# From expert output to first projections: copies, squares and first step in halves, stacks in number order

## The chip, the cores and the metric

The kernel runs on one core of a Trainium2 chip. The metric is device time in microseconds for one execution; the median of three runs of the kernel before is 797.98 us (796.89 to 799.02). The engines are TensorE (PE; its weight loads are listed as PEld), VectorE (DVE), ScalarE (ACT), GpSimd (POOL) and SyncE (SP), which here issues nearly all DMAs. Each works through its own queue in order, and they wait for each other on semaphores.

## The reference

Three layers follow each other: attention with pooled queries, a soft mixture of experts over the 2304 tokens, and a gated feed-forward layer with an RMS norm.

```python
# layer 2: 8 experts of 4 slots (n_slots = 32)
logits = x @ phi
slot_input = (softmax of logits over tokens).T @ x
for e in range(E):
    slot_out[e] = np.maximum(slot_input[e] @ w1[e], 0.0) @ w2[e]
c = softmax of logits over slots
x = c @ slot_out                                   # (2304, 512)
# layer 3, d_ff = 1536
rms = np.sqrt(np.mean(x * x, axis=-1, keepdims=True) + 1e-06)
xn = x / rms * rms_g
g = xn @ w_gate
out = (g * (1.0 / (1.0 + np.exp(-g))) * (xn @ w_val)) @ w_out
```

## The kernel before

The span of 794.3 us falls into attention (to about 545 us), the experts (to about 597 us), a short change-over (to about 619 us) and the last layer (to the end). The change lies in the change-over, and in the end of each of the two expert groups.

**Why there is a change-over.** The output of layer 2 has rank 32: each token is a mix `c` of 32 slot outputs. So the kernel never forms x. It multiplies the 32 slot outputs (scaled by rms_g) with w_gate and w_val once, to two 32 x 1536 matrices, and projects tokens from their 32 shares. A token's square sum is found from the 32 x 32 Gram matrix of the slot outputs.

**The expert output.** For each of two groups of four experts (loop over `g`), the second products gather in the bank `o_ps`; ACT copies the 128 x 512 result to `so_sb` (L1638, `o_out`), and PE transposes it in four pieces (`slot_transposes`, L1448). Two matmuls that only keep PE at work (`keep_clock`, L1432) are queued between them for the last group. DVE makes `st_plain` (L1757) and `st_scaled` (L1761); PE makes the Gram matrix.

**The squares.** PE multiplies the Gram matrix with the transposed shares `comb_t`: 512 columns (L1559) and 64 columns (L1560), then one signal `yt_ready`. DVE multiplies the 576 columns with `comb_t` into `product` (L1774). PE has `share(0, 1)` between, and then sums over slots in five pieces of 128 tokens (L1564, ten records). DVE scales to the mean (L1777), ACT takes the root (L1666), DVE the reciprocal `tok_a` (L1779).

**Shares and projections.** Tokens lie in five chunks: four of 512 and one of 256 (four tails of 64). `prescale(n)` (L1267) multiplies the shares of a chunk with `tok_a`; chunks 0 and 1 are made by DVE (`PROD_BY_DVE = 2`), 2, 3 and 4 by POOL. `share_transposes(n)` (PE, L1281) transposes four tiles of it into a PSUM bank, `shares_high(n)` (ACT, L1287) writes the rounded high part to `plain_t`, and `shares_low(n)` (DVE, L1292) subtracts it on the rows of the low part. `share(m, c)` (PE, L1515) is one quarter of slot outputs times w_gate (m = 0) or w_val (m = 1), and waits for the DMA of that quarter. After four quarters `high_half(m)` (ACT, L1655) and `low_half(m)` (DVE, L1770) split the result, and eight stacks `stack_share(k)` (PE, two matmuls, L1530 and L1532; k = 0 to 3 gate, 4 to 7 value) put it in a form of 128 rows. Two PSUM banks alternate between stacks; `share_out(k)` copies one out, 384 columns, on DVE (L1784) for k = 0, 4, 3 and on ACT (L1651) for the others. The stacks are issued in the order 0, 1, 4, 5, 2, 3, 6, 7. A projection is one matmul of 512 columns, `gate(n, f)` (L1541) or `value(n, f)` (L1545).

**The last layer.** It has 5 chunks x 12 tiles of d_ff = 60 steps. In a step, ACT takes Silu of the gate bank (L1663), DVE multiplies it with the value bank (`hid2`, L1813), ACT rounds that to `h_hi` (L1710), DVE takes the rest `h_lo` (L1818), and PE, after the projections of two steps ahead, issues 12 matmuls of 512 columns (L1617). In the first steps ACT also rounds w_out (`wo_high`, L1646) and POOL makes its low part (L1737), after it made the first high part itself (L1728).

**What sets the order.** The order on each engine is written out by hand: PE's list of `share`, `share_transposes`, `stack_share`, `gate` and `value` calls ahead of the step loop, ACT's and DVE's lists ahead of theirs. On ACT, one Silu of a single element (`warm`, L1669) after `shares_high(0)` loads the Silu table early. On SP the DMAs of w_gate, w_val and w_out are issued in this order right behind those of the experts' weights; no wait of SP stands on anything in the change-over.

Of the kernel before, what the change touches and what calls it, by code (L numbers as in the profile page):

```python
# [7 lines left out]
P = 128  # L8
FP32 = mybir.dt.float32
# [921 lines left out]
def rest(nc, mem, att, w_gate, w_val, w_out, out):  # L931
# [320 lines left out]
    prod_done, prod_rest, ct_ready = sem("prod_done"), sem("prod_rest"), sem("ct_ready")  # L1252
# [4 lines left out]
    PROD_BY_DVE = 2  # L1257

    def prescale(ops, n):
# [7 lines left out]
        return ops.tensor_tensor(dst, src.unsqueeze(2).broadcast_to(shape),  # L1267
                                 inv.unsqueeze(2).unsqueeze(3).broadcast_to(shape), ALU.mult)

    def share_transposes(pe, n):  # L1270

        bank = CT_BANK[n]
        if n < PROD_BY_DVE:
            pe.wait_ge(prod_done, n + 1)
        else:
            pe.wait_ge(prod_rest, n + 1 - PROD_BY_DVE)
# [53 lines left out]
    yt_ps = banks[:, 2:4, :]  # L1330
# [15 lines left out]
    used, stored = sem("used"), sem("stored")  # L1346
    SHARES = [(m, j) for m in range(2) for j in range(4)]
# [18 lines left out]
    PIECES_BY_DVE = (0, 4, 3)  # L1366

    def pieces_out(place):
        by_dve = sum(k in PIECES_BY_DVE for k in STACK_ORDER[:place + 1])
        return by_dve, place + 1 - by_dve  # L1370
# [53 lines left out]
    def _(pe):  # L1424
# [18 lines left out]
        def slot_transposes(g):  # L1443
            pe.wait_ge(o_out, g + 1)
            if g:
                pe.wait_ge(st_out, g)
            for c in range(KT):
                last = nc.tensor.transpose(st_ps[:, P * c:P * c + P], so_sb[:, P * c:P * c + P], ident[:])  # L1448
            last.then_inc(st_ready, 1)

        for g in range(NG):
# [31 lines left out]
            if g:  # L1483
                pe.wait_ge(o_out, g)
# [36 lines left out]
        def stack_share(k):  # L1521
# [3 lines left out]
            if stack_place(k) >= 2:  # L1525
                by_dve, by_act = pieces_out(stack_place(k) - 2)
                pe.wait_ge(wl_out_v, by_dve)
                if by_act:
                    pe.wait_ge(wl_out_a, by_act)
# [29 lines left out]
        nc.tensor.matmul(yt_ps[:, 0, :], gram[:], comb_t[:, 0:N], start=True, stop=True)  # L1559
        nc.tensor.matmul(yt_ps[:, 1, 0:TAIL], gram[:], comb_t[:, N:SQ], start=True, stop=True).then_inc(yt_ready, 1)  # L1560
        share(0, 1)
        pe.wait_ge(product_done, 1)
        for i in range(NI):
# [61 lines left out]
    def _(act):  # L1625
# [292 lines left out]
```

## Time and profile before

| | us |
|---|---|
| median of 3 runs (lowest to highest) | 797.98 (796.89 to 799.02) |
| the profiled execution | 796.09 |
| its span, from first to last instruction | 794.3 |
| PE busy | 777.4 (98%) |
| DVE busy | 465.2 (59%) |
| ACT busy | 461.8 (58%) |
| POOL busy | 182.0 (23%) |
| granted TensorE clock, mean | 0.998 of full |

The profile is of one execution, and all times in it are counted from the start of its span. PE's instructions are pipelined: the next starts before the one ahead has ended, so the text reckons a matmul's cost on PE from start to next start, and its delay for others from its start to the start of what waits for it. The same holds, by a smaller overlap, for ACT and DVE.

### The profile page before, as it was taken

To read this page: it belongs to the slowest core of one execution; us is meant where nothing else is said; L and a number is where in the kernel's file an instruction comes from. 1 tells how busy PE (TensorE), PEld (TensorE's weight loads), DVE (VectorE), ACT (ScalarE), POOL (GpSimd) and SP (SyncE) were. 2 spreads that over 40 slices of the span, in tenths; PEclk is the share of its full clock that TensorE was granted. 3 is DMA by queue.
4 is the path that set the end of the run, shared out by engine and by line. 5 is a ranking of instruction groups with operands and counts; after the bars stand their busy time and mean duration, and the time that the engine had idled before them with its cause. 6 is when DMAs were issued, how large, how long until landed. Compare 5 with 4: busy or idle time off the path is not lost.

```text
span 794.3 us, 16113 instructions
## 1 busy us (share of the span) xinstructions
PE 777.4 (98%) x5255; PEld 581.0 (73%) x5255; DVE 465.2 (59%) x895; ACT 461.8 (58%) x871; POOL 182.0 (23%) x244
## 2 busy tenths in 40 slices
PE   7999999999999999999999999999988999999998
PEld 7777777777777777777777777667324788888886
DVE  6767667666676666766666666654414545454443
ACT  5767676766767676767676676653104644343433
POOL 5351431513315233152241421000003420000000
PEclk9999999999999999999999999999999999999999
DMA  8539746374473653836538335949999001010101
GB/s 228 130 80 282 211 120 161 80 177 100 108 177 76 163 110 98 192 72 152 119 89 208 73 77 131 339 135 360 347 392 401 10 1 54 0 54 1 54 40 40
DMA packets 83030, 112.01 MB, mean 141 GB/s; under 512 B 45360, under 2 KB 47408, under 8 KB 82480
## 3 DMA queue, kind: packets, MB, share of 16 engines
q1 hardware_dynamic: 82832, 111.24, 49.3%
q8 instruction: 24, 0.39, 0.2%
q10 hardware_dynamic: 160, 0.26, 0.1%
q14 instruction: 14, 0.11, 0.0%
HBM read 71.37 MB, written 4.72 MB: 96 GB/s over the span
## 4 chain that ended last, share of the span: by engine, by line
PE 89%; SPq 4%; DMA 3%; POOL 2%; DVE 1%; issue 1%; ACT 0%; POOLq 0%; DVEq 0%; ACTq 0%
PE banks L521 23%; PE banks L584 20%; PE banks L617 19%; PE banks L1617 18%; SPq L1398 2%; PE banks L1541 2%; DMA weights<-in_moe_w 2%; PE banks L1545 2%; PE banks L1063 1%; DMA q_in<-in_q 1%; PE banks L1117 1%; PE banks L1082 1%; PE banks L1515 0%; PE banks L1468 0%; SPq L322 0%
## 5 line engine op out<-in xcount | busy, mean ns | idle before, releaser
L584 PE MATMUL banks<-k_stack,q_stack 128*128 128x384 f32 x960 | 274.8, 376 | 2.5 <-DVE q_stack L801 2.0
L772 ACT COPY pt<-banks 128x384 f32<-128x384 f32 x288 | 138.3, 480 | 152.9 <-PE banks L521 152.8
L521 PE MATMUL banks<-ident,probs 128*128 128x128 f32 x1296 | 219.6, 278 | 0.4 <-ACT probs L744 0.3
L521 PEld LDWEIGHTS banks<-ident,probs 128*128 128x128 f32 x1296 | 156.5, 140 | 67.7 <-issue 42.0
L744 ACT ACTIVATE probs<-banks,neg_max 128x1152 f32<-128x1152 f32 x144 | 175.9, 1222 | 7.4 <-DVE neg_max L841 3.0
L617 PE MATMUL banks<-pt,v_in 128*64 128x320 f32 (+1 forms) x1152 | 167.3, 417 | 0.9 <-ACT o_t L759 0.9
L584 PEld LDWEIGHTS banks<-k_stack,q_stack 128*128 128x128 f32 x960 | 147.4, 191 | 3.4 <-ACT k_stack L388 2.2
L837 DVE TENSOR_REDUCE row_max<-banks 128x1 f32<-128x384 f32 x144 | 80.1, 556 | 117.0 <-PE banks L584 115.4
L830 DVE TENSOR_REDUCE row_max<-banks 128x1 f32<-128x768 f32 x144 | 136.7, 949 | 1.7 <-PE banks L584 1.1
L617 PEld LDWEIGHTS banks<-pt,v_in 128*64 128x64 f32 x1152 | 72.0, 136 | 58.2 <-issue 25.9
L892 DVE COPY pt<-banks 128x384 f32<-128x384 f32 x144 | 80.3, 558 | 37.0 <-PE banks L521 34.3
L353 POOL TENSOR_TENSOR k_hi<-k_lo,one 128x512 fp32r<-128x512 f32 (+1 forms) x45 | 37.1, 826 | 279.7 <-ACT k_lo L690 262.3
L1617 PE MATMUL banks<-wo_hi,h_hi 128*128 128x512 f32 x216 | 84.5, 391 | 0.2 <-DVE h_lo L1818 0.2
L1617 PE MATMUL banks<-wo_lo,h_hi 128*128 128x512 f32 x216 | 84.2, 390 | 0.0
L1617 PE MATMUL banks<-wo_hi,h_lo 128*128 128x512 f32 x216 | 84.1, 389 | 0.0
L1813 DVE TENSOR_TENSOR hid<-silu,banks 128x512 f32<-128x512 f32 (+1 forms) x60 | 38.0, 633 | 40.7 <-ACT silu L1663 40.1
L1818 DVE TENSOR_TENSOR h_lo<-hid,h_hi 128x512 fp32r<-128x512 f32 (+1 forms) x60 | 38.4, 639 | 38.1 <-ACT h_hi L1710 38.1
L1710 ACT CAST h_hi<-hid 128x512 fp32r<-128x512 f32 (+1 forms) x60 | 34.7, 578 | 42.9 <-DVE hid L1813 42.9
L1663 ACT ACTIVATE silu<-banks 128x512 f32<-128x512 f32 (+1 forms) x60 | 33.3, 554 | 38.6 <-PE banks L1541 38.6
L1617 PEld LDWEIGHTS banks<-wo_hi,h_hi 128*128 128x128 f32 x216 | 40.5, 188 | 9.0 <-issue 0.7
L1617 PEld LDWEIGHTS banks<-wo_hi,h_lo 128*128 128x128 f32 x216 | 40.6, 188 | 8.5
L1617 PEld LDWEIGHTS banks<-wo_lo,h_hi 128*128 128x128 f32 x216 | 40.6, 188 | 7.9
(188 smaller groups left out, 663.3 us busy)
## 6 DMA issues: line engine op xcount, KB each, us to landing
weights<-in_moe_w SPq DMA_DIRECT2D x7, 2048.0 KB, 11.4
v_in<-in_v SPq DMA_DIRECT2D x16, 576.0 KB, 4.0
k_in<-in_k SPq DMA_DIRECT2D x30, 288.0 KB, 4.9
k_stack<-k_hi SPq DMA_DIRECT2D x30, 288.0 KB, 3.6
k_stack<-k_lo SPq DMA_DIRECT2D x30, 288.0 KB, 3.5
q_in<-in_q SPq DMA_DIRECT2D x14, 512.0 KB, 4.9
slots_of_four<-in_moe_w SPq DMA_DIRECT2D x12, 512.0 KB, 10.8
q_stack<-q_hi SPq DMA_DIRECT2D x30, 144.0 KB, 3.3
```

What stands on the lines that cost most here:

```text
L353: last = ops.tensor_tensor(high[:, cols], low[:, cols].bitcast(FP32), one[:, :].broadcast_to([P, cols.stop - cols.start]), ALU.mult)
L521: last = nc.tensor.transpose(tbank[:, bank, cols], src, ident[0:rows, 0:rows])
L584: last = nc.tensor.matmul(scores[:, bank, 0:CH], q_stack[at.par][:, h, order, cols], k_stack[at.par][:, h, keys], start=(x == 0), stop=(x ...
L617: last = nc.tensor.matmul(obank[rows, 0:GROUP_WIDTH[group]], v_in[:, par, h, D * kt:D * kt + D], pt[group][:, h, kt, :], start=(kt == 0), ...
L744: nc.scalar.activation(probs[:, odd, :].rearrange("p (c k) -> p c k", c=3), scores[:, first:first + 3, 0:CH], ACT.Exp, bias=neg_max[:, odd ...
L772: nc.scalar.copy(pt_out(at, e), pt_from(at, e)).then_inc(out_by_act, 1)
L830: nc.vector.tensor_reduce(row_max[:, odd, 0:1], scores[:, first:first + 2, 0:CH], axis=AX.XY, op=ALU.max).then_inc(partial_max, 1)
L837: nc.vector.tensor_reduce(row_max[:, odd, 1:2], scores[:, 2, 0:CH], axis=AX.X, op=ALU.max).then_inc(partial_max, 1)
L892: nc.vector.tensor_copy(pt_out(at, e), pt_from(at, e)).then_inc(out_by_dve, 1)
L1617: last = nc.tensor.matmul(y_ps[:, t, :], a[:, f % 3, cols], w[:, f, :], start=(f == 0 and x == 0), stop=(f == NFT - 1 and x == 2))
L1813: nc.vector.tensor_tensor(hid2[:, f % 2, 0:width], silu[:, f % 2, 0:width], gv_ps[:, f % 2, 1, 0:width], ALU.mult).then_inc(hid_done, 1)
L1818: nc.vector.tensor_tensor(h_lo[:, f % 3, 0:width], hid2[:, f % 2, 0:width], h_hi[:, f % 3, 0:width].bitcast(FP32), ALU.subtract).then_inc( ...
```

## The change

It has these parts:

- ACT copies each group's expert output in two pieces of 256 columns, and PE transposes the first two tiles after the first.
- The Gram product comes in parts of 384 and 192 columns, in banks 2 and 3, each with its own signal; DVE's product follows in the same parts, and the last two of the five sums wait for the second.
- All five `prescale` run on DVE, spread through its list; POOL has none.
- The one-element Silu stands right behind the root on ACT, ahead of `high_half(0)`.
- The stacks go in number order, even ones copied out by ACT, odd ones by DVE; stacks 2 and 3 come ahead of `share(1, 3)`, and `share(1, 0)` ahead of `share_transposes(1)`.
- In the first step Silu, product, high and low parts are done in halves of 256 columns; the first matmuls of the step wait for the first low half. The first Silu stands ahead of `shares_high(2)`, the second ahead of `high_half(1)` instead of in the loop; `share_out(7)` moves from ACT to DVE, behind the halves, and `share_out(3)` on DVE to ahead of `shares_low(3)`.

```diff
-    PROD_BY_DVE = 2
-    def prescale(ops, n):
+    def prescale(n):
...
-        return ops.tensor_tensor(dst, src.unsqueeze(2).broadcast_to(shape),
+        nc.vector.tensor_tensor(dst, src.unsqueeze(2).broadcast_to(shape),
...
-    yt_ps = banks[:, 2:4, :]
+    SQ_PARTS = ((2, 0, 3 * P), (3, 3 * P, SQ))
+    HALVES = (slice(0, N // 2), slice(N // 2, N))
-    STACK_ORDER = (0, 1, 4, 5, 2, 3, 6, 7)
-    PIECES_BY_DVE = (0, 4, 3)
+    def pieces_out(k):
+        return (k + 1) // 2, k // 2 + 1
...
         def slot_transposes(g):
-            pe.wait_ge(o_out, g + 1)
...
+                if c % 2 == 0:
+                    pe.wait_ge(o_out, 2 * g + c // 2 + 1)
...
-            if stack_place(k) >= 2:
-                by_dve, by_act = pieces_out(stack_place(k) - 2)
...
+            if k >= 2:
+                pe.wait_ge(wl_out_v if k % 2 else wl_out_a, k // 2)
...
         share(0, 0)
         pe.wait_ge(gram_step, 1)
         pe.wait_ge(cb_out, 1)
-        nc.tensor.matmul(yt_ps[:, 0, :], gram[:], comb_t[:, 0:N], start=True, stop=True)
-        nc.tensor.matmul(yt_ps[:, 1, 0:TAIL], gram[:], comb_t[:, N:SQ], start=True, stop=True).then_inc(yt_ready, 1)
+        for bank, first, end in SQ_PARTS:
+            nc.tensor.matmul(banks[:, bank, 0:end - first], gram[:], comb_t[:, first:end], start=True, stop=True
+                             ).then_inc(yt_ready, 1)
         share(0, 1)
-        pe.wait_ge(product_done, 1)
         for i in range(NI):
+            pe.wait_ge(product_done, 1 + (i >= 3))
...
         share(0, 2)
         share(0, 3)
         share_transposes(pe, 0)
+        share(1, 0)
         pe.wait_ge(mean_done, 1)
         share_transposes(pe, 1)
-        share(1, 0)
         stack_share(0)
         stack_share(1)
+        share(1, 1)
+        pe.wait_ge(wl_out_a, 1)
+        gate(0, 0)
         share_transposes(pe, 2)
-        share(1, 1)
-        pe.wait_ge(wl_out_v, 1)
-        gate(0, 0)
+        stack_share(2)
+        share(1, 2)
         share_transposes(pe, 3)
-        share(1, 2)
         pe.wait_ge(comb_low, 3)
         gate(0, 1)
+        stack_share(3)
         share_transposes(pe, 4)
         share(1, 3)
         stack_share(4)
         stack_share(5)
-        pe.wait_ge(wl_out_v, 2)
+        pe.wait_ge(wl_out_a, 3)
         pe.wait_ge(comb_low, CHUNKS)
         value(0, 0)
-        stack_share(2)
-        stack_share(3)
+        stack_share(6)
         value(0, 1)
-        stack_share(6)
         stack_share(7)
...
-                pe.wait_ge(lo_done, NFT * n + f + 1)
+                if k_of(n, f):
+                    pe.wait_ge(lo_done, NFT * n + f + 1)
+                else:
+                    pe.wait_ge(first_lo, 1)
                 for t in range(tiles_of(n)):
                     if k_of(n, f) == 0 and t >= 2:
+                        pe.wait_ge(lo_done, 1)
...
-            nc.scalar.copy(so_sb[:, 0:512], o_ps[:, :]).then_inc(o_out, 1)
+            for half in range(2):
+                cols = slice(2 * P * half, 2 * P * half + 2 * P)
+                nc.scalar.copy(so_sb[:, cols], o_ps[:, cols]).then_inc(o_out, 1)
...
         nc.scalar.activation(tok_b[:], tok_b[:], ACT.Sqrt, bias=eps[:, 0:1]).then_inc(root, 1)
+        nc.scalar.activation(warm[:, 1:2], ident[:, 0:1], ACT.Silu)
         high_half(0)
         shares_high(act, 0)
-        nc.scalar.activation(warm[:, 1:2], ident[:, 0:1], ACT.Silu)
+        share_out(0)
         shares_high(act, 1)
-        share_out(1)
+        act.wait_ge(gate_ready, 1)
+        for cols, done in zip(HALVES, (first_silu, silu_done)):
+            nc.scalar.activation(silu[:, 0, cols], gv_ps[:, 0, 0, cols], ACT.Silu).then_inc(done, 1)
         shares_high(act, 2)
-        gate_silu(0)
+        share_out(2)
         shares_high(act, 3)
         shares_high(act, 4)
+        gate_silu(1)
         high_half(1)
-        share_out(5)
-        share_out(2)
+        share_out(4)
...
                 if k == 0:
+                    for cols, ready, done in zip(HALVES, (first_hid, hid_done), (first_hi, hi_done)):
+                        act.wait_ge(ready, 1)
+                        nc.scalar.copy(h_hi[:, 0, cols], hid2[:, 0, cols]).then_inc(done, 1)
                     share_out(6)
-                    share_out(7)
...
-        for n in range(PROD_BY_DVE, CHUNKS):
-            prescale(nc.gpsimd, n).then_inc(prod_rest, 1)
...
-        for n in range(PROD_BY_DVE):
-            prescale(nc.vector, n).then_inc(prod_done, 1)
+        prescale(0)
+        prescale(1)
         low_half(0)
         shares_low(dve, 0)
-        share_out(0)
-        for n in range(1, CHUNKS):
-            shares_low(dve, n)
+        prescale(2)
+        share_out(1)
+        shares_low(dve, 1)
+        prescale(3)
+        shares_low(dve, 2)
+        prescale(4)
+        share_out(3)
+        shares_low(dve, 3)
+        shares_low(dve, 4)
         low_half(1)
-        share_out(4)
+        share_out(5)
+
+        def first_step():
+            dve.wait_ge(val_ready, 1)
+            for cols, ready, done in zip(HALVES, (first_silu, silu_done), (first_hid, hid_done)):
+                dve.wait_ge(ready, 1)
+                nc.vector.tensor_tensor(hid2[:, 0, cols], silu[:, 0, cols], gv_ps[:, 0, 1, cols], ALU.mult
+                                        ).then_inc(done, 1)
+            for cols, ready, done in zip(HALVES, (first_hi, hi_done), (first_lo, lo_done)):
+                dve.wait_ge(ready, 1)
+                nc.vector.tensor_tensor(h_lo[:, 0, cols], hid2[:, 0, cols], h_hi[:, 0, cols].bitcast(FP32), ALU.subtract
+                                        ).then_inc(done, 1)
+            share_out(7)
...
-                if k == 0:
-                    share_out(3)
```

## Rows read from the trace of the kernel before

**Rows 1.** Page, chain that ended last, share of the span by engine.
```profile
PE 89%; SPq 4%; DMA 3%; POOL 2%; DVE 1%; issue 1%; ACT 0%; POOLq 0%; DVEq 0%; ACTq 0%
```

**Rows 2.** Timeline of ACT: start us, us, engine, line, operation, out<-in, count, idle before.
```profile
559.90 0.65 ACT L1169 COPY z_sum<-banks 128x256 f32<-128x256 f32 x2 [5.04 <-PE banks L1117]
...
597.45 0.58 ACT L1638 COPY hid<-banks 128x512 f32<-128x512 f32 x1 [11.74 <-PE banks L1505]
```

**Rows 3.** Timeline of PE, 601 to 603 us, columns as in rows 2.
```profile
601.42 0.85 PE L1515 MATMUL banks<-w_gv,st_scaled 128*32 128x384 f32 x8
602.41 1.28 PE L1564 MATMUL banks<-row_group,product 128*128 128x4 f32 x10
```

**Rows 4.** Source line L1267: ns min/median/max, first and last start us, forms.
```profile
L1267 POOL TENSOR_TENSOR shares<-comb,tok_a x3: 1029/1493/1553, 604.6 to 607.6; 128x512 f32<-128x512 f32 x2, 64x512 f32<-64x512 f32 x1
L1267 DVE TENSOR_TENSOR shares<-comb,tok_a x2: 691/1114/1537, 604.6 to 605.2; 128x512 f32<-128x512 f32 x2
```

**Rows 5.** Timeline of ACT, 603 to 609 us.
```profile
603.94 0.31 ACT L1666 ACTIVATE tok_b<-tok_b,eps 128x20 f32<-128x20 f32 x1 [4.39 <-DVE tok_b L1777]
605.18 0.48 ACT L1655 CAST w_hi<-banks 128x384 fp32r<-128x384 f32 x1 [0.93 <-PE banks L1515]
...
606.64 1.28 ACT L1669 ACT_TABLE_LOAD   x1
...
608.04 0.57 ACT L1287 CAST plain_t<-banks 128x512 fp32r<-128x512 f32 x1
```

**Rows 6.** Timeline of PE, 605 to 613 us.
```profile
605.34 0.66 PE L1281 MATMUL banks<-ident,shares 128*128 128x128 f32 x4 [0.22 <-DVE shares L1267]
606.89 0.63 PE L1281 MATMUL banks<-ident,shares 128*128 128x128 f32 x4 [0.89 <-DVE shares L1267]
...
608.23 0.45 PE L1530 MATMUL banks<-w_hi,spread 128*128 128x384 f32 x1
...
609.04 0.60 PE L1281 MATMUL banks<-ident,shares 128*128 128x128 f32 x4
609.57 0.85 PE L1515 MATMUL banks<-w_gv,st_scaled 128*32 128x384 f32 x8
610.35 0.50 PE L1541 MATMUL banks<-plain_t,w_low 128*128 128x512 f32 x1
610.68 0.60 PE L1281 MATMUL banks<-ident,shares 128*128 128x128 f32 x4
...
612.43 0.46 PE L1281 MATMUL banks<-ident,shares 64*128 64x64 f32 x4
612.82 0.85 PE L1515 MATMUL banks<-w_gv,st_scaled 128*32 128x384 f32 x8
```

**Rows 7.** Timeline of PE, 614 to 617 us.
```profile
614.86 0.45 PE L1530 MATMUL banks<-w_hi,spread 128*128 128x384 f32 x1 [1.19 <-DVE w_lo L1770]
...
616.13 0.50 PE L1545 MATMUL banks<-plain_t,w_low 128*128 128x512 f32 x1 [0.30 <-DVE w_low L1784]
```

**Rows 8.** Timeline of DVE, 613 to 617 us.
```profile
613.33 0.43 DVE L1292 TENSOR_TENSOR plain_t<-banks,plain_t 64x256 fp32r<-64x256 f32 x1 [0.64 <-ACT plain_t L1287]
...
615.51 0.56 DVE L1784 CAST w_low<-banks 128x384 fp32r<-128x384 f32 x1 [0.71 <-PE banks L1532]
616.73 0.69 DVE L1813 TENSOR_TENSOR hid<-silu,banks 128x512 f32<-128x512 f32 x1 [0.66 <-PE banks L1545]
```

**Rows 9.** Timeline of PE, 625 to 629 us.
```profile
625.64 0.39 PE L1617 MATMUL banks<-wo_hi,h_hi 128*128 128x512 f32 x1
...
628.82 0.39 PE L1617 MATMUL banks<-wo_hi,h_hi 128*128 128x512 f32 x1
```

**Rows 10.** Tile w_gv: DMA issues ns min/median/max, first and last start us; landing.
```profile
L1408 SPq DMA_DIRECT2D w_gv<-in_moe_w_val x4: 552/593/636, 588.8 to 590.7; - x4
...
DMA to landing us min/median/max: 12.2/15.4/19.8
```

**Rows 11.** Timeline of POOL, 613 to 616 us.
```profile
614.40 1.28 POOL L1737 TENSOR_TENSOR wo_lo<-wo_raw,wo_hi 128x512 fp32r<-128x512 f32 x1
```

More of the change, by code:

```diff
@@ L1250, in rest @@
     wo_raw = mem.sb("wo_raw", [P, NFT, DM], FP32)
-    prod_done, prod_rest, ct_ready = sem("prod_done"), sem("prod_rest"), sem("ct_ready")
+    prod_done, ct_ready = sem("prod_done"), sem("ct_ready")
     comb_high, comb_low = sem("comb_high"), sem("comb_low")
@@ L1346, in rest @@
     used, stored = sem("used"), sem("stored")
+    first_silu, first_hid, first_hi, first_lo = sem("first_silu"), sem("first_hid"), sem("first_hi"), sem("first_lo")
+    HALVES = (slice(0, N // 2), slice(N // 2, N))
     SHARES = [(m, j) for m in range(2) for j in range(4)]
@@ L1356, in tiles_of @@
         return width_of(n) // P
-    STACK_ORDER = (0, 1, 4, 5, 2, 3, 6, 7)
-    def stack_place(k):
-        return STACK_ORDER.index(k)
     def k_of(n, f):
         return NFT * n + f
-    PIECES_BY_DVE = (0, 4, 3)
-    def pieces_out(place):
-        by_dve = sum(k in PIECES_BY_DVE for k in STACK_ORDER[:place + 1])
-        return by_dve, place + 1 - by_dve
+    def pieces_out(k):
+        return (k + 1) // 2, k // 2 + 1
     o_rows = out.rearrange("(b s) d -> b s d", b=B)
@@ L1483, in _ @@
             if g:
-                pe.wait_ge(o_out, g)
+                pe.wait_ge(o_out, 2 * g)
             if g == 0:
@@ L1649, in share_out @@
             m, j = SHARES[k]
-            act.wait_ge(wl_ready, stack_place(k) + 1)
+            act.wait_ge(wl_ready, k + 1)
             nc.scalar.copy(w_low[:, m, QW * j:QW * j + QW], tb3[:, k % 2, 0:QW]).then_inc(wl_out_a, 1)
@@ L1705, in _ @@
                 k = NFT * n + f
-                if k >= 1:
+                if k >= 2:
                     gate_silu(k)
-                act.wait_ge(hid_done, k + 1)
-                halves_free(n, f)
-                nc.scalar.copy(h_hi[:, f % 3, 0:width], hid2[:, f % 2, 0:width]).then_inc(hi_done, 1)
                 if k == 0:
+                    for cols, ready, done in zip(HALVES, (first_hid, hid_done), (first_hi, hi_done)):
+                        act.wait_ge(ready, 1)
+                        nc.scalar.copy(h_hi[:, 0, cols], hid2[:, 0, cols]).then_inc(done, 1)
                     share_out(6)
-                    share_out(7)
+                else:
+                    act.wait_ge(hid_done, k + 1)
+                    halves_free(n, f)
+                    nc.scalar.copy(h_hi[:, f % 3, 0:width], hid2[:, f % 2, 0:width]).then_inc(hi_done, 1)
                 if n == 0 and f + 1 < NFT:
@@ L1771, in low_half @@
                                     ALU.subtract).then_inc(share_lo, 1)
-        dve.wait_ge(yt_ready, 1)
-        nc.vector.tensor_tensor(product[:, 0:SQ], yt_ps.rearrange("p a n -> p (a n)")[:, 0:SQ], comb_t[:],
-                                ALU.mult).then_inc(product_done, 1)
+        for n, (bank, first, end) in enumerate(SQ_PARTS):
+            dve.wait_ge(yt_ready, n + 1)
+            nc.vector.tensor_tensor(product[:, first:end], banks[:, bank, 0:end - first], comb_t[:, first:end],
+                                    ALU.mult).then_inc(product_done, 1)
         dve.wait_ge(sq_ready, 1)
@@ L1782, in share_out @@
             m, j = SHARES[k]
-            dve.wait_ge(wl_ready, stack_place(k) + 1)
+            dve.wait_ge(wl_ready, k + 1)
             nc.vector.tensor_copy(w_low[:, m, QW * j:QW * j + QW], tb3[:, k % 2, 0:QW]).then_inc(wl_out_v, 1)
@@ L1808, in _ @@
                 k = NFT * n + f
+                if k == 0:
+                    first_step()
+                    continue
                 dve.wait_ge(silu_done, k + 1)
```

10 lines of the change are left out of this document (2 added, 8 removed).

## The prediction

> **What bounds the kernel now.** I read the page's chain first: 89% of it is PE [rows 1]. So only places where PE waits, or where its queue is in a worse order, can give time. The timelines of ACT, DVE and PE around the change-over show them.
>
> Before it, PE waits for expert weights; the output copy then takes 0.58 us of ACT alone (597.45). An ACT pair of 256 columns elsewhere takes 0.65 together, 0.37 each with overlap [rows 2]. `share(0,1)` starts at 601.42 and holds PE for 0.78 (the pitch of a share, part 2), so PE is free at 602.20, but the squares start at 602.41 [rows 3]. Then `prescale`: of DVE's two, at 604.6 and 605.2, one takes 0.69, the other 1.54, as long as POOL's (1.49 and 1.55), which run at the same time [rows 4]. ACT's root ends at 604.25, `high_half(0)` starts at 605.18, and the Silu table takes 1.40 from its start to the next copy [rows 5]. PE sat idle 0.89 us before `share_transposes(1)` at 606.89, because of the long `prescale`. `share(1,3)` starts at 612.82 [rows 6]. Stack 4 follows at 614.86 and `value(0,0)` at 616.13, with PE idle 1.19 and 0.30 us before them [rows 7]. DVE copies the piece for it (0.56 us) and starts `hid2` at 616.73 [rows 8]. From 625.64 on the steps come every 3.18 us (to 628.82) [rows 9]; I use 3.17. That is PE's own work, and nothing of the change touches it. The change's worth is therefore the shift of the matmuls that start at 625.64.
>
> **Part 1, up to the root: 0.41 us.** Halved, the output copy gives its first half after 0.37 instead of 0.58: 0.21 gained, as PE can do two transposes while ACT does the rest; I take 0.20. It is nothing if PE is held by the clock-keeping matmuls in front. For group 0 the earlier copy ends in a wait for weights: nothing. The Gram product keeps its 576 columns; its second signal comes when the only one came. DVE's product now starts some 0.3 us earlier, on 384 columns, so the squares can start when `share(0,1)` is through, 0.21 earlier; no more, since that share stands ahead of them in PE's queue. Sum 0.41 (bounds 0.2 and 0.6). `share_transposes(0)` goes from 605.34 to 604.93 [rows 6].
>
> **Part 2, PE's run from there.** I add pitches of rows 6: `share` 0.78 (609.57 to 610.35); transposes 0.53 (609.04 to 609.57), 0.56 for the first, 0.39 for the tails (612.43 to 612.82); `gate` 0.33 (610.35 to 610.68); two stacks 0.81 (608.23 to 609.04), one 0.40. In the new order: transposes(0) 604.93, share(1,0) 605.49, transposes(1) 606.27, stacks 0, 1 606.80, share(1,1) 607.61, gate(0,0) 608.39, transposes(2) 608.72, stack 2 609.25, share(1,2) 609.65, transposes(3) 610.43, gate(0,1) 610.96, stack 3 611.29, transposes(4) 611.69, share(1,3) 612.08. That is 0.74 earlier than 612.82, although two stacks (0.80) more stand ahead of it: 0.41 is part 1, and the 0.89 stall is gone.
>
> What must be ready in time:
>
> - `prescale` on DVE. With POOL silent I take 0.69 for each, 0.65 from start to start. The second then ends at 605.5 and transposes(1) needs it at 606.27. The bound above is 1.54.
> - The Silu table beside the root: root ends 604.25 - 0.41 = 603.84, plus 1.40 gives `high_half(0)` at 605.24 instead of as early as 604.8. Its copy (0.48) and DVE's low half (0.55) end at 606.30; PE reaches stack 0 at 606.80. Hidden with 0.5 to spare. In its old place the table ran while the second transposes were awaited, but held `shares_high(1)` some 0.5 us too; that goes.
> - DVE's queue: low_half(0) 605.75, shares_low(0) 606.30 (0.69 each), prescale(2) to 607.64, share_out(1) 607.80, shares_low(1) 608.50 (after ACT, which does share_out(0) at 607.45 first), prescale(3) to 609.84 (PE needs it at 610.43), shares_low(2) 610.19 to 610.88 (ACT's two Silu halves stand ahead of its high part; PE needs it at 610.96), prescale(4) to 611.53 (needed 611.69), share_out(3), shares_low(3), shares_low(4) to 613.55. DVE is thus as full as PE here, with 0.1 to 0.2 us to spare in two places.
> - The DMAs of w_val: the last is issued at 590.7 and lands 19.8 later, at 610.5; share(1,3) comes at 612.08 [rows 10].
>
> A page of the Trainium skill speaks against the table's new place: "ScalarE: Activation LUTs", section What ACT_TABLE_LOAD costs, adds a drain of about 1.38 us to the load of 1.28, for every switch. The trace has 1.28 for the load and the next copy 1.40 after its start, so no drain behind it; rows decide. By the page, an estimate: high_half(0) at 606.6, stack 0 at 607.7, and 0.9 us less gained.
>
> **Part 3, from share(1,3) to value(0,0).** Before, 2.04 us from share(1,3) to stack 4 [rows 6, 7]. Silu(1) now stands ahead of `high_half(1)`; it ends 0.05 after the share is ready. So stack 4 starts at 612.08 + 2.04 + 0.05 = 614.17, 0.69 earlier. From there to value(0,0) 1.27 before; ACT's copy (0.48) in place of DVE's (0.56) makes it 1.19: 615.36, against 616.13 before.
>
> **Part 4, the first step in halves.** DVE started 0.60 after value(0,0): now 615.96. A half of 256 columns takes 0.43 on DVE [rows 8] and 0.37 on ACT. Product A to 616.39, B to 616.78. ACT's high A to 616.79, B to 617.18. DVE's low A from 616.82 to 617.25. gate(0,2) needs product B: 616.82, value(0,2) 0.33 later, and the first step's matmuls 0.23 after that, at 617.38; low A, ready at 617.29, is just hidden. Low B (617.64) and the last two pieces, copied by 618.1, are needed only at 618.8 and later. The second step's low part, by the same additions, is ready at 620.2 and needed at 620.6. So no stall follows, and step 2 starts at 617.38 + 2 x 3.17 = 623.72, against 625.64: **1.9 us gained**. POOL's first low part of w_out ends at 615.68 [rows 11] and hangs on its DMA, not on this work; the step needs it at 617.38. It keeps 1.7 us to spare.
>
> The shared port is a point where the rule tells more than the row. "SBUF — State Buffer", section Who interferes with whom, says that a DVE instruction with two SBUF inputs and a GpSimd one that reads SBUF block each other for a whole instruction. That favours 0.69 for a `prescale` alone; it also lets POOL's second low part of w_out hold the second `h_lo` on DVE, for about 0.1 us here by the times above, which is hidden.
>
> **Sum.** 796.09 of the profiled execution minus 1.9 is 794.2. This execution lies 1.9 below the median of the runs (797.98) and just under their lowest (796.89), so what I forecast is a difference: median **796.1 us**.
>
> **The rivals.**
>
> - A, the forecast: 796.1, own range 795.3 to 797.0 (part 1 from 0.2 to 0.6; pitches 0.05 off over some ten places). Chance 0.58.
> - B, PE's run packs tighter: inside a run stacks may cost 0.35, the refill of some 0.1 behind a share goes, and the root is up to 0.3 earlier if DVE's smaller product also helps. DVE's full queue speaks against. Gain 2.6: 795.4. Chance 0.16.
> - C, the Silu table: a drain in front of or behind it that the old place hid. 0.9 less: 797.0. Against it: 1.40 in rows 5. Chance 0.05.
> - D, DVE or ACT is the bound from share_out(1) on: hand-offs of 0.05 to 0.1 more at each of the alternating places make gate(0,1), prescale(4) and low_half(1) late, and the two stacks put ahead of share(1,3) cost their 0.8 without return, with 0.1 for the waits: 797.0. The spare times of 0.1 speak for it, the hand-offs in the trace (0.03 to 0.04) against. Chance 0.13.
> - E, slower: `prescale` is slow by itself from the second on (1.54, with its broadcast inputs), not because of POOL. Then three more stand on DVE at 0.85 too much, the fourth already was there: prescale(2) ends at 608.9, (3) at 611.6, (4) at 613.7, transposes(4) start at 613.8, share(1,3) at 614.2, stack 4 at 616.2 instead of 614.17, 2.1 later: 798.2, 0.2 over before. It decides from 1.48 us per `prescale` on. For it: one of DVE's two did take that long. Against: the first, with the same inputs, took 0.69. Chance 0.08.
>
> A measurement of this kernel can tell about 0.3%, 2.4 us, from no change. Faster by more than that: B and the upper edge of A with the spread of the runs, 0.33. Slower by more: only E with such a spread, 0.05. The rest, 0.62, lies within. The range runs from 795.0 to 797.9: it takes in B, C and D and leaves out E and the far ends.
>
> **What would show it.** Right in part 1: the squares start about 0.4 earlier, straight behind `share(0,1)`. In part 2: five `prescale` of about 0.69 on DVE, no stall of PE over 0.2 between transposes(0) and share(1,3), and that share about 0.7 earlier. In part 3: stack 4 to value(0,0) in 1.2. In part 4: the first step's matmuls 2.0 after value(0,0), no wait before the second step, and the third step 1.9 earlier. The forecast is wrong if a `prescale` takes over 1 us, if the copy behind the table load starts more than 1.5 after it, if gate(0,1) waits for DVE's low parts or stack 4 for DVE's queue rather than for the share, or if the first step waits for w_out.

## The result, and the profile after

The changed kernel takes 795.36 us (median of 8 runs, 792.95 to 796.07), the kernel before in the same comparison 797.42 (8 runs, 796.4 to 799.02): a ratio of 0.9968, with a 95% interval of 0.9956 to 0.9981. That is 0.32% faster, and clear of no change. The quotient of the two medians is 0.9974, a difference of 2.06 us; the ratio on record lies nearer to that of the means (795.05 and 797.50). The forecast was 796.1 us, with 0.62 on "within 0.3%": the mechanism came as forecast, the call that the gain can't be told from no change did not.

The page of the profiled execution (span; busy time by engine; the chain that ended last):

```profile
span 794.1 us, 16115 instructions
...
PE 777.9 (98%) x5255; PEld 581.1 (73%) x5255; DVE 467.0 (59%) x902; ACT 461.7 (58%) x874; POOL 178.5 (22%) x241
...
PE 93%; SPq 2%; DMA 2%; DVE 1%; issue 1%; ACT 1%
```

The span is 794.1 us and was 794.3: by this one pair of executions next to nothing is gained. Where the gain went is seen ahead of the change-over. Timeline of PE in the changed kernel:

```profile
595.87 3.23 PE L1498 MATMUL banks<-weights,hid_t 128*32 128x512 f32 x16 [3.29 <-DMA weights<-in_moe_w]
...
599.90 0.60 PE L1441 MATMUL banks<-ident,hid 128*128 128x128 f32 x4
...
603.10 0.85 PE L1508 MATMUL banks<-w_gv,st_scaled 128*32 128x384 f32 x8
603.88 1.28 PE L1555 MATMUL banks<-row_group,product 128*128 128x4 f32 x10
...
606.81 0.66 PE L1277 MATMUL banks<-ident,shares 128*128 128x128 f32 x4 [0.23 <-DVE shares L1266]
...
608.18 0.66 PE L1277 MATMUL banks<-ident,shares 128*128 128x128 f32 x4
...
613.87 0.85 PE L1508 MATMUL banks<-w_gv,st_scaled 128*32 128x384 f32 x8
615.91 0.44 PE L1520 MATMUL banks<-w_hi,spread 128*128 128x384 f32 x1 [1.19 <-DVE w_lo L1771]
...
617.10 0.50 PE L1535 MATMUL banks<-plain_t,w_low 128*128 128x512 f32 x1 [0.22 <-ACT w_low L1648]
...
619.10 0.47 PE L1612 MATMUL banks<-wo_hi,h_hi 128*128 128x512 f32 x1
```

```profile
625.55 0.39 PE L1612 MATMUL banks<-wo_hi,h_hi 128*128 128x512 f32 x1
```

The same 16 matmuls in the kernel before:

```profile
595.40 1.92 PE L1505 MATMUL banks<-weights,hid_t 128*32 128x512 f32 x16 [2.65 <-DMA weights<-in_moe_w]
```

PE waited 3.29 us for the last weights (2.65 before), and then its 16 matmuls took 3.23 us, where before they took 1.92. The work by stretches, where the last number but two is the granted clock as a share of full speed:

```profile
590.00:596.00 6.00, 2.71 (x30) 0.68 (x24) 0.00 (x0) 0.00 (x0) 0.00 (x0) 1.00 1.05 406
596.00:598.00 2.00, 2.00 (x13) 0.42 (x12) 0.00 (x0) 0.00 (x0) 0.00 (x0) 0.59 1.00 412
598.00:600.00 2.00, 2.00 (x11) 0.75 (x4) 0.00 (x0) 0.79 (x3) 0.00 (x0) 0.56 1.03 424
600.00:602.00 2.00, 1.91 (x48) 1.09 (x46) 0.81 (x3) 1.35 (x2) 0.00 (x0) 1.00 1.00 412
```

From 596 to 600 us the granted clock was 0.59 and 0.56: for most of that time it was at its lower level, 1.2 of 2.4 GHz, after PE had idled. ACT's copy starts 1.75 us later than before (599.20, against 597.45 in [rows 2]): 0.47 of that is the later landing of the weights, nearly all the rest the slower matmuls. Counted from that copy, the matmuls of the third step start 28.19 us later in the kernel before [rows 2, 9] and 26.35 us later here: 1.84 us are gained, all inside the change-over. From the third step to the end the two profiles, like the twelve others, take the same 168.6 us.

ACT and DVE there, and the five `prescale` as a source line (ns min/median/max); last, the reciprocal of the kernel before:

```profile
599.20 0.65 ACT L1635 COPY hid<-banks 128x256 f32<-128x256 f32 x2 [13.65 <-PE banks L1498]
...
605.41 0.31 ACT L1663 ACTIVATE tok_b<-tok_b,eps 128x20 f32<-128x20 f32 x1 [4.05 <-DVE tok_b L1779]
605.74 1.28 ACT L1664 ACT_TABLE_LOAD   x1
...
607.14 0.46 ACT L1652 CAST w_hi<-banks 128x384 fp32r<-128x384 f32 x1
```

```profile
605.75 0.28 DVE L1781 RECIPROCAL tok_a<-tok_b 128x20 f32<-128x20 f32 x1 [0.38 <-ACT tok_b L1663]
606.06 1.29 DVE L1266 TENSOR_TENSOR shares<-comb,tok_a 128x512 f32<-128x512 f32 x2
...
617.63 0.75 DVE L1817 TENSOR_TENSOR hid<-silu,banks 128x256 f32<-128x256 f32 x2 [0.16 <-PE banks L1535]
618.52 0.76 DVE L1821 TENSOR_TENSOR h_lo<-hid,h_hi 128x256 fp32r<-128x256 f32 x2
```

```profile
L1266 DVE TENSOR_TENSOR shares<-comb,tok_a x5: 684/693/694, 606.1 to 612.7; 128x512 f32<-128x512 f32 x4, 64x512 f32<-64x512 f32 x1
```

```profile
604.28 0.28 DVE L1779 RECIPROCAL tok_a<-tok_b 128x20 f32<-128x20 f32 x1 [0.38 <-ACT tok_b L1666]
```

These rows show: the copy in two halves (0.65 for both); the squares right behind `share(0,1)` (603.10 and 0.78 later 603.88, where before PE stood idle 0.21 [rows 3]); all five `prescale` at 0.68 to 0.69, where the second took 1.54 [rows 4]; the load of the Silu table from 605.74 and `high_half(0)` at 607.14, 1.40 later, as in [rows 5], so nothing more is waited for behind the load; `share_transposes(1)` 1.37 behind the first, not 1.55 [rows 6]; and product and low part of the first step in halves.

### The profile page after: what moved, and what is told of

Read it like the earlier page. It is cut to its first block, busy times and chain, and to the rows that moved or that the text cites. A ratio compares the mean times of both kernels' runs of the same rounds, so it can differ in the third digit from the quotient of the medians.

```text
span 794.1 us, 16115 instructions
## 1 busy us (share of the span) xinstructions
PE 777.9 (98%) x5255; PEld 581.1 (73%) x5255; DVE 467.0 (59%) x902; ACT 461.7 (58%) x874; POOL 178.5 (22%) x241
## 4 chain that ended last, share of the span: by engine, by line
PE 93%; SPq 2%; DMA 2%; DVE 1%; issue 1%; ACT 1%
PE banks L521 24%; PE banks L584 21%; PE banks L617 20%; PE banks L1612 18%; SPq L1390 2%; PE banks L1531 2%; PE banks L1535 2%; DMA weights<-in_moe_w 1%; PE banks L1063 1%; DMA q_in<-in_q 1%; PE banks L1117 1%; PE banks L1082 1%; PE banks L651 1%; PE banks L1508 0%; PE banks L1461 0%
```

## The experiments

The kernels with "fill" in their name, and stacks_old_again, hold PE's clock with three filling matmuls (the edit of fill_wait). Times are of the change-over's three stretches in each profile: from ACT's first output copy to DVE's `st_plain` copy, from there to DVE's reciprocal, and from the reciprocal to the first matmul of the third step.

| kernel | copy to st_plain | to reciprocal | to third step | median us | ratio to before (95%) |
|---|---|---|---|---|---|
| before | 1.33 | 5.50 | 21.36 | 797.42 | |
| changed | 1.34 (slow clock) | 5.21 | 19.80 | 795.36 | 0.9968 (0.9956 to 0.9981) |
| prescale_on_pool | 1.95 (slow clock) | 5.21 | 19.96 | 796.8 | 0.9983 (0.9968 to 0.9997) |
| table_old_place | 1.18 | 5.21 | 19.82 | 794.96 | 0.9964 (0.9948 to 0.998) |
| first_step_whole | 1.60 (slow clock) | 5.28 | 20.51 | 796.75 | 0.9986 (0.9969 to 1.0003) |
| fill_wait | 1.18 | 5.21 | 19.80 | 794.48 | 0.9959 (0.9945 to 0.9974) |
| before_fill | 1.33 | 5.48 | 21.40 | 797.04 | 0.9983 (0.996 to 1.0006) |
| part1_whole_fill | 1.40 | 5.50 | 19.79 | 794.65 | 0.9953 (0.993 to 0.9976) |
| stacks_old_order_fill | 1.18 | 5.21 | 22.44 (slow clock) | 795.98 | 0.9972 (0.9949 to 0.9994) |
| before_prescale_dve_fill | 1.34 | 5.47 | 20.93 | 796.3 | 0.9976 (0.9954 to 0.9999) |
| after_again | 1.18 | 5.22 | 19.79 | 795.74 | 0.9973 (0.9955 to 0.9992) |
| fill_again | 1.19 | 5.21 | 19.80 | 794.34 | 0.9966 (0.9953 to 0.9979) |
| stacks_old_again | 1.18 | 5.21 | 20.43 | 795.04 | 0.9974 (0.9961 to 0.9986) |
| share_early_fill | 1.18 | 5.21 | 20.14 | 794.22 | 0.9958 (0.9944 to 0.9972) |

Where nothing disturbs them the stretches repeat within 0.04 us, while medians of one kernel move by 0.1 to 0.9 us (794.48 and 794.34 with the fill; 795.36 and 795.74 changed; 795.98 and 795.04 for stacks_old_order_fill and stacks_old_again, which are one kernel); so parts of 0.2 to 0.7 us are read from the stretches. Each stretch is of one execution.

**prescale_on_pool**

```diff
+        for n in (2, 3, 4):
+            prescale(n, nc.gpsimd, prod_rest)
...
-        prescale(2)
...
-        prescale(3)
...
-        prescale(4)
```

> The changed kernel with one part undone: prescale(2), (3) and (4) on POOL again, started there right behind the reciprocal. The measure, C, is the length of the change-over in the trace, from ACT's first copy of the last expert output to the first matmul of the third step: 28.19 us before, 26.34 after. Theory (the port is shared, the new order hides it): DVE's second prescale takes about 1.54 again instead of 0.65, but PE reaches transposes(1) only when share(1,0) is through, so at most 0.2 is lost there, and DVE is rid of three operations: C 26.2 to 26.6, the time within 0.3 us of the changed kernel. Rival (the move to DVE is what carries the gain): C longer by 0.8 or more, 27.2.

Timelines of DVE and of POOL:

```profile
606.40 2.15 DVE L1267 TENSOR_TENSOR shares<-comb,tok_a 128x512 f32<-128x512 f32 x2
608.47 0.54 DVE L1777 TENSOR_TENSOR w_lo<-banks,w_hi 128x384 fp32r<-128x384 f32 x1
```

```profile
606.44 4.01 POOL L1267 TENSOR_TENSOR shares<-comb,tok_a 128x512 f32<-128x512 f32 x3 [125.01 <-DVE tok_a L1787]
```

DVE's two took 2.15 together again (1.29 alone, above), so it is POOL at the same time that makes the second slow; rival E is out. The last stretch grew by 0.16 only, as the theory has it. C was 27.12, outside the theory's 26.2 to 26.6 and near the rival's 27.2, but 0.77 us of it came from the clock in the first stretch (1.95 against 1.18 at whole clock): C was a poor measure, and the stretches took its place. The median is 1.4 us above the changed kernel's, not within the 0.3 expected; the two come from two comparisons whose intervals overlap, and don't decide it.

**table_old_place**

```diff
-        nc.scalar.activation(warm[:, 1:2], ident[:, 0:1], ACT.Silu)
         high_half(0)
         shares_high(act, 0)
+        nc.scalar.activation(warm[:, 1:2], ident[:, 0:1], ACT.Silu)
```

> The changed kernel with the one-element Silu behind shares_high(0) again. Theory (the table load is hidden in either place; share_out(0) comes 0.3 later but PE needs it only then): C 26.3 to 26.5. Rival (the new place matters, because the load in the old one holds the copies that gate(0,0) and shares_low(1) wait for): C 26.7 or more. Second rival (the new place costs, since DVE waits 0.28 for w_hi): C 26.1.

19.82 against 19.80: the move of the table is worth nothing. Rival C is out too. (C came out at 26.21, under the 26.3 to 26.5 expected, because the 26.34 it started from held a first stretch at the slow clock; fill_wait has 26.19.)

**first_step_whole**

```diff
-    HALVES = (slice(0, N // 2), slice(N // 2, N))
+    HALVES = (slice(0, N),)
```

> The changed kernel with the first step's Silu, product, high and low part each in one piece of 512 columns; the rest as changed. Theory: the chain product 0.69, high 0.62, low 0.69 with two hand-offs ends 0.65 later than low half A does now, and PE waits for it: C 26.9 to 27.1, time 0.6 us longer. Rival (gate(0,2) and value(0,2) hide the chain anyway): C 26.4.

Timeline of PE, `value(0,2)` and the first step behind it:

```profile
618.41 0.40 PE L1535 MATMUL banks<-plain_t,w_low 128*128 128x512 f32 x1
619.54 0.47 PE L1612 MATMUL banks<-wo_hi,h_hi 128*128 128x512 f32 x1 [0.73 <-DVE h_lo L1821]
```

PE waits 0.73 us for the low part, and the stretch is 0.71 longer (0.65 expected). C was 27.39, over the 27.1 expected, again with the slow clock in the first stretch (1.60). The halves are the largest single part that was undone.

**fill_wait**

```diff
                     if f == 2:
                         group_transposes()
+                    if f == 6:
+                        for _ in range(3):
+                            nc.tensor.matmul(h_ps[:, 0, :], ident[:], hid_t[:, 0:4, :].rearrange("p f q -> p (f q)"),
+                                             start=True, stop=True)
                     pe.wait_ge(w2_in[f // 2], 64)
```

> The changed kernel with three matmuls of 512 columns (fp32, result unused) put in the place where PE waits for the last quarter of the second group's w2. In the profiled execution of the changed kernel PE idled 3.29 us there, the granted clock was then 0.59 and 0.56 for 4 us, and the 16 last matmuls took 3.23 us; before, PE idled 2.65 us, the clock stayed 1.00 and they took 1.92. Theory (that drop is what differs between executions of either kernel and hides part of the gain): the 16 matmuls take 1.92 in the profile, the clock stays 1.00 from 590 to 602 us, C stays 26.3, and the median falls by 0.3 to 1.3 us against the changed kernel. Rival (the spread of the times comes from elsewhere, as the start or the landing of the weights): the median does not move, or rises by up to 0.3 where the weights land before the three are through.

PE's timeline around the wait, and the stretches behind it:

```profile
591.37 2.84 PE L1492 MATMUL banks<-hid_t,ident 128*128 128x512 f32 x6
594.54 1.92 PE L1502 MATMUL banks<-weights,hid_t 128*32 128x512 f32 x16 [0.33 <-DMA weights<-in_moe_w]
```

```profile
594.00:596.00 2.00, 1.67 (x17) 0.42 (x16) 0.00 (x0) 0.00 (x0) 0.00 (x0) 1.00 1.02 418
596.00:598.00 2.00, 1.95 (x16) 0.97 (x8) 0.22 (x1) 1.39 (x3) 0.00 (x0) 1.00 1.02 418
598.00:600.00 2.00, 1.95 (x43) 1.06 (x44) 0.58 (x2) 0.74 (x2) 0.00 (x0) 1.00 1.02 418
```

The three fillers take 2.84 us, the wait shrinks to 0.33, the clock stays whole and the 16 matmuls take 1.92. The median is 0.88 below the changed kernel's, in another comparison. In all eight profiles with the fill these 16 took 1.92; of the six profiles of kernels without it, only that of the kernel before shows 1.92, the others 2.56 to 3.54.

**before_fill**

```diff
+                    if f == 6:
+                        for _ in range(3):
+                            nc.tensor.matmul(h_ps[:, 0, :], ident[:], ...)
```

> The kernel before with the three filling matmuls of the run fill_wait and nothing else. From here on every kernel has them, so that the clock of the change-over is whole, and three stretches are read: from ACT's first output copy to DVE's st_plain copy (1.33 us before, 1.18 in fill_wait), from there to the reciprocal (5.50 and 5.21), and from the reciprocal to the third step's first matmul (21.36 and 19.80). Theory (the fill takes away what idle PE costs, in either kernel): 1.33, 5.50, 21.36 again; the granted clock stays at 1.00; the median falls by about 1 us against before, and fill_wait stays some 2.0 us below this run. Rival (the fill helps only the changed kernel): no fall.

1.33, 5.48, 21.40, and clock 1.00. The median is 0.64 below before in its own comparison, but the ratio's interval (0.996 to 1.0006) holds no change, so the fall is not shown. What shows more is the spread: the standard deviation of its 12 runs is 0.65 us, against 1.5 for before in that comparison (leaving out one run of 806.87; 2.1 with it). With whole clock the change is worth 0.15 + 0.27 + 1.60 = 2.02 us by the stretches; the medians of before_fill and fill_wait differ by 2.6, from two comparisons, and their ratios by 0.24%, 1.9 us.

**part1_whole_fill**

```diff
-            for half in range(2):
...
+            nc.scalar.copy(so_sb[:, 0:512], o_ps[:, :]).then_inc(o_out, 2)
-    SQ_PARTS = ((2, 0, 3 * P), (3, 3 * P, SQ))
+    SQ_PARTS = ((2, 0, N), (3, N, SQ))
```

and one product of 576 columns on DVE.

> fill_wait with the output copy, the Gram product and its squares whole again (512 and 64 columns, one signal), the rest as changed. Theory: 1.33, 5.50 and 19.8, so 0.44 us longer than fill_wait. Rival (the halves only move a wait): 1.2 to 1.3 and 5.2 to 5.3.

1.40, 5.50, 19.79: 0.50 us come back, 0.44 expected (the first stretch is 0.07 longer than in the kernel before). The median (794.65, 0.17 above fill_wait's) can't tell so small a part.

**stacks_old_order_fill** and, once more, **stacks_old_again**

```diff
         share_transposes(pe, 2)
-        stack_share(2)
         share(1, 2)
...
         gate(0, 1)
-        stack_share(3)
...
         value(0, 0)
+        stack_share(2)
+        stack_share(3)
-        stack_share(6)
         value(0, 1)
+        stack_share(6)
```

> fill_wait with the stacks in the order 0, 1, 4, 5, 2, 3, 6, 7 again: stack 2 and 3 between value(0,0) and value(0,1), their copies behind; even ones still on ACT, odd ones on DVE. Theory (DVE's list, not PE's, holds share(1,3), so the two stacks ahead of it cost nothing there and save their 0.7 us behind it): the last stretch 20.3 to 20.6 instead of 19.80. Rival D of the prediction (the two stacks delay share(1,3) by their 0.8): 19.6 to 19.8.

The first profile can't be compared in the last stretch: PE waited 0.84 us for w_gate and w_val, and behind `share(1,3)`, where it idles, the clock fell. Stretches of that run, granted clock last but two:

```profile
612.00:614.00 2.00, 1.22 (x12) 0.45 (x12) 1.28 (x3) 1.29 (x3) 0.00 (x0) 1.00 1.05 385
614.00:616.00 2.00, 1.59 (x5) 1.16 (x5) 0.35 (x1) 0.48 (x1) 1.38 (x2) 0.63 0.66 239
616.00:618.00 2.00, 2.00 (x6) 1.79 (x7) 1.31 (x3) 0.61 (x2) 0.93 (x1) 0.52 0.18 62
618.00:620.00 2.00, 1.97 (x9) 1.50 (x9) 1.93 (x5) 1.48 (x4) 0.28 (x1) 1.00 0.03 12
```

> stacks_old_order_fill, once more, since in its profile the granted clock fell between 614 and 618 us and the gate and value DMAs came 0.8 us late for PE, so that its last stretch (22.44) can't be compared. Theory: without both, 20.3 to 20.6, and the median again 1.0 to 1.5 us above fill_wait's, of which 0.6 is the order and the rest a clock that falls more often where PE idles behind share(1,3). Rival D: 19.6 to 19.8.

PE in the second run:

```profile
610.96 0.49 PE L1537 MATMUL banks<-plain_t,w_low 128*128 128x512 f32 x1 [0.15 <-DVE plain_t L1288]
611.67 0.46 PE L1277 MATMUL banks<-ident,shares 64*128 64x64 f32 x4 [0.22 <-DVE shares L1266]
612.06 0.85 PE L1514 MATMUL banks<-w_gv,st_scaled 128*32 128x384 f32 x8
614.10 0.44 PE L1526 MATMUL banks<-w_hi,spread 128*128 128x384 f32 x1 [1.19 <-DVE w_lo L1777]
```

The last stretch is 20.43, so the order is worth 0.63. The reciprocal starts at 604.00 there, so `share(1,3)` comes 8.06 us behind it; with two more stacks ahead of it, in the changed kernel, 8.12 (605.75 to 613.87). The two stacks cost 0.06 of their 0.8, and rival D is out: without them PE waits for DVE, 0.15 us before `gate(0,1)` and 0.22 before the tail transposes. The median lies 0.7 above fill_again's, on the same chip, and 0.56 above fill_wait's, not the 1.0 to 1.5 expected.

**before_prescale_dve_fill**

```diff
-    PROD_BY_DVE = 2
+    PROD_BY_DVE = 5
         shares_low(dve, 0)
+        prescale(nc.vector, 2).then_inc(prod_done, 1)
         share_out(0)
```

and the fourth and fifth behind `shares_low(1)` and `shares_low(2)`.

> The kernel before with the fill and with one part of the change done alone: all five prescale on DVE, the third behind shares_low(0), the fourth behind shares_low(1), the fifth behind shares_low(2). Theory (the collision with POOL held transposes(1) by 0.9, and of that 0.65 reaches share(1,3)): the last stretch 20.6 to 20.9 instead of 21.36. Rival (with its ACT list as before, the table load holds shares_high(1), and the three operations more on DVE eat the gain): 21.2 or more.

20.93, against 21.40 in before_fill: 0.47 gained, 0.42 less than the stall of 0.89 and just outside what I expected. PE there:

```profile
611.16 0.66 PE L1281 MATMUL banks<-ident,shares 128*128 128x128 f32 x4 [0.17 <-DVE shares L1267]
```

Counted from the reciprocal (605.28) PE is 0.86 us ahead of before_fill up to `gate(0,0)` (610.50); then `share_transposes(3)` starts 0.66 behind that gate instead of 0.33, because it waits for the fourth `prescale` on DVE. That one stands behind `shares_low(1)`, and this behind ACT's `shares_high(1)`, which in the old order comes after the table load.

**after_again** and **fill_again**, on one chip (no edit; the fill alone).

> The changed kernel itself, once more, beside the next run on one chip, to part two sources of its gain. Theory: the last stretch (reciprocal to the third step's first matmul) is 19.80 again; the time lies about 2 us below before where the clock holds, and the idle wait for the weights costs it on average 0.5 to 1 us against the next run.

> fill_wait, once more. Theory (the wait for the weights lets the clock fall in many executions of the changed kernel, in none with the fill): the 16 last matmuls of the experts take 1.92 us and the median is 0.5 to 1.0 us below after_again. Rival (the difference of 0.9 between the two medians so far was chance): within 0.2 us.

The medians are 795.74 and 794.34, 1.4 us apart, more than the 1.0 I allowed; the standard deviations 1.84 and 0.71. The 16 matmuls in the trace of after_again:

```profile
594.28 3.54 PE L1498 MATMUL banks<-weights,hid_t 128*32 128x512 f32 x16 [2.53 <-DMA weights<-in_moe_w]
```

They took 3.54 us, nearly twice the time, though PE had idled only 2.53 us, less than the 2.65 after which the clock stayed whole in the kernel before. So the length of this one wait does not by itself decide whether the clock falls.

**share_early_fill**

```diff
         gate(0, 1)
+        share(1, 3)
         stack_share(3)
         share_transposes(pe, 4)
-        share(1, 3)
```

with `high_half(1)` ahead of `shares_high(4)` on ACT, and `low_half(1)` ahead of `share_out(3)` and `shares_low(4)` on DVE.

> A version past the change: fill_wait with share(1,3) ahead of stack 3 and share_transposes(4) on PE, high_half(1) ahead of shares_high(4) on ACT, and on DVE low_half(1) ahead of share_out(3) and shares_low(4). PE idled 1.19 us behind share(1,3), for ACT's high and DVE's low half; now the stack, the tail transposes and DVE's other work lie there. Theory: stack 4 starts 0.85 earlier and all behind it follows: the last stretch 18.9 to 19.1 instead of 19.80, the median 0.8 us below fill_again. Rival (DVE's queue is full, and what is moved behind low_half(1) makes value(0,0) wait for shares_low(4)): 19.6 or more.

Timelines of PE, DVE and POOL:

```profile
612.74 0.45 PE L1524 MATMUL banks<-w_hi,spread 128*128 128x384 f32 x1 [0.26 <-DVE w_lo L1775]
...
613.93 0.50 PE L1539 MATMUL banks<-plain_t,w_low 128*128 128x512 f32 x1
...
615.62 0.39 PE L1539 MATMUL banks<-plain_t,w_low 128*128 128x512 f32 x1
616.97 0.50 PE L1616 MATMUL banks<-wo_hi,h_hi 128*128 128x512 f32 x1 [0.96 <-POOL wo_lo L1742]
```

```profile
615.36 1.83 DVE L1825 TENSOR_TENSOR h_lo<-hid,h_hi 128x256 fp32r<-128x256 f32 x2
```

```profile
614.20 1.04 POOL L1733 TENSOR_TENSOR wo_hi<-wo_raw,one_col 128x512 fp32r<-128x512 f32 x1 [133.82 <-DMA wo_raw<-in_moe_w_out]
615.38 2.98 POOL L1742 TENSOR_TENSOR wo_lo<-wo_raw,wo_hi 128x512 fp32r<-128x512 f32 x2
```

The idle 1.19 us behind `share(1,3)` shrank to 0.26, and `value(0,0)` starts 10.62 us behind the reciprocal (603.31) instead of 11.35. Then PE waits 0.96 us for POOL's first low part of w_out, and DVE's two halves of `h_lo` take 1.83 instead of 0.76, while POOL works on SBUF at the same time. The last stretch is 20.14, and the median 0.12 below fill_again: no gain that can be told. The test is not clean: w_out's first piece landed late in this execution (POOL starts on it at 614.20, 10.89 us behind the reciprocal; in fill_wait at 612.58, 9.60 behind). Without the wait the stretch would be 19.18, an estimate from 20.14 less 0.96, and near what was expected; whether this order gains stays open. fill_wait and share_early_fill have the lowest medians; which of them is better is not shown.

## Why the prediction was wrong

Its steps held. By the three stretches at whole clock (fill_wait for the first):

| part | forecast gain us | measured |
|---|---|---|
| 1, output copy | 0.20 | 0.15 |
| 1, squares | 0.21 | 0.29 |
| 2, reciprocal to share(1,3) | 8.54 - 8.21 = 0.33 | 8.54 - 8.12 = 0.42 |
| 3, share(1,3) to value(0,0) | 0.03 | 3.31 - 3.23 = 0.08 |
| 4, value(0,0) to the third step | 1.15 | 9.51 - 8.45 = 1.06 |
| sum | 1.92 | 2.00 |

- Part 1, "the squares can start when `share(0,1)` is through": so it is. "It is nothing if PE is held by the clock-keeping matmuls" did not happen at whole clock.
- Part 2, PE's run: from transposes(0) to share(1,3) it took 7.06 us (606.81 to 613.87) against 7.15 in the forecast; the 0.69 of a `prescale` without POOL held. DVE's list was as full as said: undoing the stack order shows that PE had the room for two stacks.
- Part 3: the Silu ahead of `high_half(1)` cost nothing; stack 4 starts 2.04 behind `share(1,3)`, as before.
- Part 4: 2.00 from `value(0,0)` to the first step, forecast 2.02. first_step_whole (0.71) and the order of the stacks (0.63) carry it, and they are the two largest parts undone. Undone one by one they make 1.34, more than the 1.06 of this part: they don't simply add up.

The step that failed is the last: "A measurement of this kernel can tell about 0.3%, 2.4 us, from no change ... The rest, 0.62, lies within." The forecast of 1.9 us was 0.24%, and I called it no change. Eight runs of each gave an interval of about 0.12% to either side, 1.0 us, and the measured 0.32% lies more than twice that away from no change. No row of the prediction carries the 0.3%; it is about the spread of the three runs at hand (2.13 us), which is the scatter of single runs, not the resolution of a comparison of medians. In size the sum is right: 1.9 us is a ratio of 0.9976, inside the measured 0.9956 to 0.9981. Even against the limit of 0.3% the outcome was close: the ratio (0.32%) lies just beyond it, the quotient of the medians (0.26%) just within.

The half microsecond between the 2.0 of the stretches and the 2.55 of the ratio is not settled. It can be chance: the interval is 1.5 to 3.5 us, and the medians themselves differ by 2.06 here and by 1.96 in the comparison of after_again and fill_again (797.70 for 32 runs of the kernel before, two of 1540 and 1948 us left out, and 795.74 for after_again). It can be the clock, which the forecast took as given. Of those 32 runs, the eight with a mean clock of at least 0.9985 have a median of 795.96 us, the seven under 0.9965 one of 798.59: 2.6 us between executions of one program, more than the whole change. But the mean does not say where the clock was low. In the profiles of four kernels, before and changed among them, it was low near the start too. The stretch from 10 to 12 us, granted clock last but two, in the kernel before and then in the changed one:

```profile
10.00:12.00 2.00, 2.00 (x11) 1.97 (x10) 1.75 (x4) 0.87 (x2) 1.85 (x5) 0.50 0.87 266
```

```profile
10.00:12.00 2.00, 2.00 (x11) 1.90 (x10) 1.65 (x4) 0.66 (x2) 1.84 (x6) 0.50 0.88 283
```

The change does not touch that place, nor the wait for weights that lets the clock fall: with the fill, what is left of that wait is 0.62 us in both profiles of the old order and 0 to 0.63 in the six of the new. It does shorten PE's idle time behind the wait (the 0.89 us of [rows 6], for one), and stacks_old_order_fill shows that the clock can fall there as well. That the changed kernel's clock falls less often is argued, not shown, and the mean clock of the 12 runs of after_again, 0.9973 against 0.9977 for the 32 of the kernel before, speaks against it.

The clock is not the only source of the scatter either. fill_wait and fill_again are one kernel, and the clock is whole in both profiles. ACT's copy of `z_sum` (the first line of [rows 2]) in the one and in the other:

```profile
558.59 0.65 ACT L1169 COPY z_sum<-banks 128x256 f32<-128x256 f32 x2 [5.04 <-PE banks L1117]
```

```profile
559.38 0.65 ACT L1169 COPY z_sum<-banks 128x256 f32<-128x256 f32 x2 [5.04 <-PE banks L1117]
```

PE's last 16 expert matmuls start at 594.54 and 596.48. Of the 1.9 us between the two spans (791.4 and 793.3), 0.79 had come up before that copy and 1.15 between it and the landing of the last weights; the change-over took 26.2 us in both.

The drain of about 1.38 us that the Trainium skill ("ScalarE: Activation LUTs", What ACT_TABLE_LOAD costs) adds to a table load shows in no run. From the load's start to the next copy it is 1.40 or 1.41 us in 13 of the 14 profiles, in both places (1.49 in stacks_old_order_fill, where w_gate came late), and the load starts within 0.02 us of the end of the instruction ahead of it. The rule of the Trainium skill on the shared port ("SBUF — State Buffer", Who interferes with whom: a VectorE instruction with two SBUF inputs and a GpSimd one that reads SBUF contend for it) agrees with three cases here: 1.54 against 0.69 before and after, 2.15 against 1.29 for two `prescale` with the other work back on POOL, 1.83 against 0.76 in share_early_fill.

## What to carry to other kernels

Add up PE's own pitches in the new order and set beside each step the time at which ACT, DVE, POOL and the DMAs are ready for it: this gave 1.92 us of a measured 2.00. Then ask what the measurement resolves with the number of runs it will have, before calling a quarter of a percent nothing. And look at the waits ahead of the stretch you change: idle time of PE can be paid for with a lower clock in the work that follows, and here three matmuls whose result nobody uses, put into the wait, were cheaper (fill_again 1.4 us under after_again).

## What the runs showed of the hardware

- Behind a wait of 2.5 to 3.4 us the granted clock fell in five of six profiles without the fill, to 0.50 to 0.57 of full in the lowest stretch of 2 us; the 16 matmuls took 2.56 to 3.54 us instead of 1.92. With three filling matmuls (2.84 us) it was whole there in eight of eight. The standard deviation of the times was 0.65 to 1.04 us in the kernels with the fill and 1.09 to 1.84 in the changed kernel and its variants without it.
- The wait that did not lower the clock (2.65 us) was longer than one that did (2.53 us).
- The clock can also fall inside the change-over: 0.63 and 0.52 from 614 to 618 us in stacks_old_order_fill, where PE had idled 0.38, 0.46, 0.22 and 1.19 us on the way; and near the start, 0.50 from 10 to 12 us, in four of 14 profiles.
- Beside POOL's work on SBUF, DVE's took longer: 0.85 us for one `prescale` (1.54 instead of 0.69), 1.07 us for the two halves of `h_lo` (1.83 instead of 0.76). Operations given to the idle POOL were a loss for DVE; what that was worth depends on the order around them, 0.47 us in the old one (before_prescale_dve_fill), 0.16 in the new (prescale_on_pool).
- One kernel's executions differ by about 2 us with the clock whole: 0.8 us of it arose before 559 us, 1.15 between there and the landing of the last weights (fill_wait and fill_again).
